# Linear attention and two expert layers on one core: the first block's four tiles scored in two pairs of batches, with quarter scores, and the last tile's state sums moved behind the first steps

## The reference, cut to what matters

```python
batch, n_heads, seq, head_dim = (4, 8, 768, 48)
for t in range(S):                         # attention, state is D x D per head
    state = alpha[:, :, t, :, None] * state + einsum('bhd,bhe->bhde', k[:, :, t], v[:, :, t])
    y[:, :, t] = einsum('bhd,bhde->bhe', q[:, :, t], state)
x = y.transpose(0, 2, 1, 3).reshape(3072, 384)
h = x @ w_in;  g = h * clip(h + 3, 0, 6) / 6;  x = g @ w_out       # 384 -> 2048 -> 384
h = x @ w_in2; g = relu(h) ** 2;               out = g @ w_out2
```

## Time and profile before

| | |
|---|---|
| median of 3 runs | 860.57 us (860.54 to 860.71) |
| the profiled execution: its time | 859.13 us |
| the profiled execution: its span | 857.4 us |
| TensorE busy | 849.5 us (99%) |
| VectorE, ScalarE, GpSimd busy | 331.1, 327.9 and 316.6 us |
| instructions | 15319 |

### The profile page before, as it was taken

The page is one execution under the profiler, slowest core; times in us unless marked ns, Lnnn a source line. Parts: engine busy times, 40 slices in busy tenths (PEclk is TensorE's granted clock), DMA queues, the critical chain, the costliest instruction groups (busy, mean ns, idle before and its releaser), DMA issues.

```text
span 857.4 us, 15319 instructions
## 1 busy us (share of the span) xinstructions
PE 849.5 (99%) x6312; PEld 703.7 (82%) x6312; DVE 331.1 (39%) x466; ACT 327.9 (38%) x586; POOL 316.6 (37%) x248
## 2 busy tenths in 40 slices
PE   8999999999999999999999999999999999999998
PEld 7888888888888888888888888888888888888886
DVE  8977545564455555421333311212211211211111
ACT  4754433343434333333445423333323333323332
POOL 2855443344433443433333333333333333333332
PEclk9999999999999999999999999999999999999999
DMA  9743233332233332200323001000000000100101
GB/s 351 296 108 96 40 95 87 90 78 72 71 81 100 86 80 75 61 16 5 111 74 111 0 1 38 1 0 26 12 1 8 29 1 0 37 1 1 37 0 39
DMA packets 67496, 51.84 MB, mean 60 GB/s; under 512 B 50785, under 2 KB 57185, under 8 KB 67425
## 3 DMA queue, kind: packets, MB, share of 16 engines
q1 hardware_dynamic: 67424, 50.84, 19.4%
HBM read 40.60 MB, written 8.26 MB: 57 GB/s over the span
## 4 chain that ended last, share of the span: by engine, by line
PE 97%; DMA 1%; SPq 0%; ACT 0%; issue 0%; ACTq 0%
PE h_ps L1046 46%; PE o_ps L1059 46%; PE att_all L939 1%; PE att_all L923 1%; DMA w_in_raw<-w_in 1%; PE att_all L990 1%; PE att_all L1014 1%; SPq L400 0%; PE h_ps L976 0%; ACT k_tok L561 0%; PE att_all L901 0%; PE att_all L976 0%; SPq L406 0%; SPq L402 0%; ACT squares L549 0%
## 5 line engine op out<-in xcount | busy, mean ns | idle before, releaser
L522 POOL TENSOR_TENSOR g_parts<-h_act,g_parts 128x512 fp32r<-128x512 f32 x192 | 257.8, 1343 | 518.9 <-ACT g_parts L603 518.8
L1059 PE MATMUL o_ps<-g_parts,w_out_hi 128*128 128x512 f32 x1152 | 327.0, 389 | 0.0
L1046 PE MATMUL h_ps<-x_parts,w_in_hi 128*128 128x512 f32 x1152 | 295.3, 392 | 0.0
L1059 PEld LDWEIGHTS o_ps<-g_parts,w_out_hi 128*128 128x128 f32 x1152 | 216.1, 188 | 45.0 <-POOL g_parts L522 0.2
L1046 PEld LDWEIGHTS h_ps<-x_parts,w_in_hi 128*128 128x128 f32 x1152 | 214.4, 188 | 45.3
L603 ACT ACTIVATE g_parts<-h_act 128x512 fp32r<-128x512 f32 x192 | 121.3, 632 | 271.4 <-PE o_ps L1059 241.5
L787 DVE SCALAR_TENSOR_TENSOR h_act<-h_ps,h_gate 128x512 f32<-128x512 f32 x96 | 66.3, 691 | 290.5 <-ACT h_gate L598 290.5
L1059 PE MATMUL o_ps<-g_parts,w_out_lo 128*128 128x512 f32 x576 | 165.6, 389 | 0.0
L1046 PE MATMUL h_ps<-x_parts,w_in_lo 128*128 128x512 f32 x576 | 161.7, 389 | 0.0
L1046 PEld LDWEIGHTS h_ps<-x_parts,w_in_lo 128*128 128x128 f32 x576 | 108.1, 188 | 22.6
L1059 PEld LDWEIGHTS o_ps<-g_parts,w_out_lo 128*128 128x128 f32 x576 | 108.1, 188 | 22.5
(11 more groups left out here) (114 smaller groups left out, 375.8 us busy)
## 6 DMA issues: line engine op xcount, KB each, us to landing
inputs<-att_in SPq DMA_DIRECT2D x18, 772.0 KB, 4.5
w_in_raw<-w_in SPq DMA_DIRECT2D x8, 768.0 KB, 7.8
w_out_raw<-w_out SPq DMA_DIRECT2D x8, 768.0 KB, 9.1
result<-inputs SPq DMA_DIRECT2D x18, 256.0 KB, 2.4
inputs<-v_in SPq DMA_DIRECT2D x20, 192.0 KB, 2.8
k_tok<-turned_keys SPq DMA_DIRECT2D x18, 192.0 KB, 2.9
x_mid<-att_in SPq DMA_DIRECT2D x4, 772.0 KB, 8.9
turned_keys<-x_mid SPq DMA_DIRECT2D x36, 64.0 KB, 2.3
```

Source lines behind the costliest of these rows:

```text
L522: nc.gpsimd.tensor_tensor(g_parts[:, g % 2, 1, :], h_act[:, g % 2, :], g_parts[:, g % 2, 0, :].bitcast(F32), ALU.subtract).then_inc(g_lo, 1)
L1046: last = nc.tensor.matmul(h_ps[g % 2][:, :], w[:, m, cols], x_parts[:, n % 2, part, m, :], start=m == 0 and i == 0, stop=m == KT - 1 and i ...
L1059: return nc.tensor.matmul(o_ps[m][:, :], w[:, f, m * P:(m + 1) * P], g_parts[:, g % 2, part, :], start=f == 0 and w is w_out_hi and part = ...
```

## The change

Only the first block's attention is changed, and the order of the work up to step 3.

- `score` writes quarters: early keys by early queries, late keys by late queries, and early keys by late queries (the "cross" part, which needs no mask). Two batches share one table: batch b of a pair goes to PSUM rows 64b to 64b + 63. A tile has 24 products of 64 columns where it had 16 of 128 (each is two instructions in the trace).
- `mask(p)` masks a pair of tiles at once with two instructions of 512 columns, one for the early quarters, one for the late ones, instead of two for each tile. ScalarE copies the cross part to SBUF (`copy_cross`).
- `attend_first(p)` multiplies a pair's values in products of 64 x 64 by 64 columns: three early shares of 8 products, six late ones.
- All four keys are scaled by GpSimd, directly after the first scan of their tile. `split_w(0)` follows on GpSimd with no wait for the queries.
- `first_state` is one copy of 112 rows instead of two of 48. The values for the state sums come as a further input, four transfers of 192 KB.
- ScalarE's `split_w(1)` moves behind the last tile's results and `copy_keys(3)`. `add_up_first(3)` moves to step 3, and `first_state(3)` too. The clearing of `state`, the full mask and the last two groups of dummy matmuls go.

```diff
-WARM_UP = (14, 8, 3, 2)
+WARM_UP = (14, 8)
 @@ SP
             load_tile(1)
+            load_tile(2)
+            load_values_to_sum(0)
+            load_tile(3)
             load_values(0)
-            load_tile(2)
             load_values(1)
-            load_tile(3)
             load_w(0)
+            load_values_to_sum(1)
+            load_values_to_sum(2)
             load_values(2)
             load_values(3)
             load_w(1)
+            load_values_to_sum(3)
 @@ GpSimd
-            for t in (1, 2):
-                pool.wait_ge(to_token_made, t + 1)
+            for t in range(BATCH):
                 scale_keys(t)
-            pool.wait_ge(q_scaled, BATCH)
             split_w(0)
             split_w(1)
 @@ ScalarE
             check_to_token(0)
-            x_high(0)
+            copy_cross(0)
+            copy_keys(1)
             first_state(0)
-            split_w(0)
-            copy_keys(1)
             check_from_end(1)
             check_to_token(1)
+            x_high(0)
             x_high(1)
+            split_w(0)
+            copy_keys(2)
             first_state(1)
-            copy_keys(2)
-            split_w(1)
-            copy_keys(3)
-            x_high(2)
+            first_state(2)
+            copy_cross(1)
             for m in range(KT):
                 last_x_high(m)
-            first_state(2)
-            first_state(3)
+            copy_keys(3)
+            split_w(1)
             check_from_end(2)
 ...
+                if g == score_at(BATCH):
+                    first_state(BATCH - 1)
 @@ VectorE
             make_decays(0)
-            scale_keys(0)
             scale_queries(0)
             make_decays(1)
+            scale_queries(1)
+            make_from_end(2)
             mask(0)
-            scale_queries(1)
-            make_decays(2)
-            mask(1)
+            make_to_token(2)
             scale_queries(2)
             make_decays(3)
-            scale_keys(3)
             scale_queries(3)
-            mask(2)
-            mask(3)
-            for t in range(BATCH - 1):
+            mask(1)
+            for t in range(2):
                 x_low(t)
 @@ TensorE
+                early, late = slice(PART, TILE), slice(0, PART)
+                for keys_of, first_query, place, signal in ((early, 0, FIRST_SCORES, None),
+                                                            (late, PART, [c + SCORES_W for c in FIRST_SCORES], scored),
+                                                            (early, PART, FIRST_CROSS, cross_scored)):
+                    ...
+                            last = nc.tensor.matmul(banks[PART * b:PART * (b + 1), col:col + PART], keys(t)[rows, j, keys_of],
+                                                    queries(t)[rows, j, first_query:first_query + PART], ...)
 ...
             warm_up(1)
-            attend_first(0)
-            add_up_first(0)
             score(1)
             turn_keys(1)
-            warm_up(2)
-            attend_first(1)
+            add_up_first(0)
+            attend_first(0)
             add_up_first(1)
             score(2)
             turn_keys(2)
-            pe.wait_ge(masked, 2)
-            warm_up(3)
             add_up_first(2)
             score(3)
+            attend_first(1)
             turn_keys(3)
-            attend_first(2)
-            attend_first(3)
-            add_up_first(3)
 ...
+                if g == score_at(BATCH):
+                    add_up_first(BATCH - 1)
```

More of the change, by code:

```diff
@@ L140, in hi_parts @@
 def hi_parts(t):
[L143 removed]
+    return t + 1 if t < 2 else 2 + KT + 2 * (t - BATCH + 1)
 def pieces_of(t):
@@ L328, in chunked_program @@
         v_loaded = [sem(f"v_loaded{i}") for i in range(BATCH + 2)]
+        vs_loaded = [sem(f"vs_loaded{i}") for i in range(BATCH)]
         w_loaded = [sem(f"w_loaded{i}") for i in range(len(W_ORDER))]
@@ L585, in first_state @@
                 act.wait_ge(u_made, t + 1)
-                act.wait_ge(state_cleared, 1)
-                for half in range(2):
-                    rows = half_rows(half)
-                    nc.scalar.activation(state[rows, t, :, :], sums(t, half), ACT.Copy).then_inc(state_made, 1)
+                nc.scalar.activation(state[:, t, :, :], first_sums(t), ACT.Copy).then_inc(state_made, 2)
             def gate(g):
@@ L896, in score @@
-                for j in range(PAIRS):
-                    for part in range(2):
-                        cols = slice(HALF * part, HALF * (part + 1))
-                        for half, bank in enumerate((bank_even, bank_odd)):
-                            rows = half_rows(half)
-                            last = nc.tensor.matmul(bank[cols, j * TILE:(j + 1) * TILE], keys(t)[rows, j, cols],
-                                                    queries(t)[rows, j, :], start=True, stop=True)
-                            if j == PAIRS - 1 and part == 1:
-                                last.then_inc(scored, 1)
+                past(pe, masked, 4 * p)
@@ new lines, in attend_first @@
+            def attend_first(p):
+                pe.wait_ge(masked, 4 * p + 2)
+                if p:
+                    pe.wait_ge(state_made, 6)
+                for m in FIRST_ORDER[p]:
+                    if p and m == 0:
+                        pe.wait_ge(cross_copied, 2)
+                    if p and m == 2:
+                        pe.wait_ge(masked, 8)
+                    share(p, m, 0, 2 * p, masked_first[:, :, 0:PAIRS, :], True)
+                pe.wait_ge(cross_copied, p + 1)
+                pe.wait_ge(masked, 4 * p + 4)
+                for m in range(KT):
+                    share(p, m, 1, 2 * p, cross_scores, True)
+                    last = share(p, m, 1, 2 * p + 1, masked_first[:, :, PAIRS:, :], False)
+                    if p and m < KT - 1:
@@ L980, in attend_first @@
                         last.then_inc(last_y_made, 1)
-                last.then_inc(y_made, 1)
+                last.then_inc(y_made, 2)
             def attend(t):
```

215 lines of the change are left out of this document (117 added, 98 removed).

## The result

The kernel after took 870.26 us (median of 6 runs, 867.79 to 871.31), the one before 860.64 us in the same sessions (6 runs, 860.54 to 861.19). The ratio is 1.0108, with a 95% interval of 1.0094 to 1.0121: slower by 9.6 us where 5.5 was forecast, and 1.7 above the range. The profiled execution has a span of 868.9 us against 857.4, so 11.5 us of difference are in the trace to be found.

The account below looks back on a forecast made before the run. The prediction took the time as the start of `hidden(0)` plus a TensorE stream without holes. Its terms, 2.9 + 2.2 + 0.4 = +5.5 us, gave 864.6 profiled, 866.1 as median, range 861.7 to 868.6.

Parts of the forecast that it names:

- parts 1 and 2: VectorE and GpSimd before `hidden(0)`: GpSimd's keys delay second scans; its first split delays tile 3's queries to 24.4, not 21.0.
- The walk of VectorE: Forecast timeline of VectorE's scans, masks and query scalings through tiles 0 to 3, tile 3's second scan ending at 20.4.
- The waiting engine wins: At the SBUF port shared by VectorE and GpSimd, GpSimd's waiting split goes before tile 3's query scaling: 3.4 us taken.
- Rival B: Tile 3's query scaling keeps its place ahead of GpSimd's split; `hidden(0)` at 25.7, median 862.7; chance 0.25.
- rival C: The VectorE-GpSimd port is no bar in these tiles; `hidden(0)` at 24.7, holes about 0, 859.5, not slower; chance 0.20.
- part 3: TensorE from tile 3's scaled queries through scores, masks, attention and turned keys: `hidden(0)` at 29.1 against 26.21, +2.9 us.
- T: The start of `hidden(0)`, the first step: 26.21 us in the kernel before, forecast 29.1.
- Rival D: TensorE idles from 20.7 to 24.5 and its clock falls; four microseconds at half rate, +1, 867.1; chance 0.10.
- Part 4: Steps behind `hidden(0)`: late `split_w(1)` delays GpSimd's second split and `low(1)`, so TensorE waits; holes of +2.2 us.
- Part 5: `add_up_first(3)` placed in step 3 adds 0.35 us and two switches of shape: +0.4 us, 0.56 at most.

Follow-up runs that it names:

- e9: Kernel before, with GpSimd no longer waiting for tile 3's query scaling ahead of its first split; 868.75 us.
- e1: Kernel after, with GpSimd's first split waiting again until all four queries are scaled; 870.61 us.
- e4: Kernel after with 3 dummy products of 512 columns ahead of `score(2)` and 11 of 128 behind `add_up_first(2)`; 871.31 us.
- e5: e2 with its 14 and 8 dummy products of 128 columns replaced by 4 and 2 of 512; 867.75 us.
- e12: e3 with 3 dummy products of 512 columns ahead of `score(2)`; 870.21 us.
- e10: Kernel before without its 3 dummy products ahead of tile 1's attention and 2 ahead of tile 2's sums; 862.25 us.
- e7: Kernel after with the loads held after tile 3's values until TensorE has turned tile 2's keys; 868.29 us.
- e2: Kernel after with ScalarE's `split_w(1)` moved early, ahead of `copy_cross(1)`; 865.99 us.
- e3: Kernel after with both the edit of e1 and that of e2; 867.22 us.
- e11: Kernel before with ScalarE's second split moved behind the state copies of tiles 2 and 3; 865.57 us.
- e16: e14 with each group's late share right behind its merged product, and nothing left out of the sums; 863.90 us.
- e8: Kernel before with its 14, 8, 3 and 2 dummy products of 128 columns replaced by 56, 32, 12 and 8 of 32; 896.10 us.
- e13: e3 with products that share weights merged: early keys against all 128 queries, early values against both parts; 864.96 us.
- e14: e2 with products that share weights merged: early keys against all 128 queries, early values against both parts; 863.98 us.

## Why the prediction was wrong

**Direction and parts 1 and 2: right in themselves.** Slower was forecast at 0.75. The walk of VectorE, the second scans of 2.1 to 2.2 us and the query scaling (23.8 to 24.4 forecast, ended 24.6) came as written. The waiting engine wins: the split made the scaling 3.74 us long in the kernel after, and in e9 two splits together made TensorE stand still for 5.5 us. Rival B's mechanism (the scaling keeps its place) and rival C (the port is no bar) are refuted by these two traces. But in the changed kernel those 3.4 us were not on the path. e1 took them away and the time stayed. So that `hidden(0)` came late was forecast from a delay that set nothing there, and this half of the right direction is luck.

**The step that failed is part 3, "from queries to T": +2.9 forecast, +6.0 measured.** It priced 48 instructions by their durations, and those held: 48 records in 1.6 us at the high clock. It had TensorE through with its own work and idle from 20.7 us, waiting for the query scaling, and did not ask where the instructions come from. 588 records stand ahead of T instead of 358, and each block of 126 waits for a packet behind a full data queue. The hole of 2.45 us at record 347 and the low clock from it on made TensorE arrive at tile 3's scores at 25.74, 1.1 us behind the scaling, and half rate took most of the rest of the way to T. The holes of e4, e5 and e12 (at 220 or 221, 346 or 347, 472 or 473, and 599 or 600), e10 (the same hole in the kernel before) and e7 (sooner packets, a shorter hole) show that it is the instruction supply. How T's 3.1 us divide between hole and clock is not shown, since what e12 saved on the clock it lost to the next packet. No rival had the supply. The rows for it existed: the packets at 15.9, 22.3 and 28.6 us in the trace of before, and a count of 358 in the earlier trace rows.

**Rival D was mis-sized.** It did happen, but at the issue hole and not in a wait for the queries. It was priced at 4 us of half rate and +1. The clock was low for some 10 us ahead of `hidden(0)`, and the work in it (rest of the scores, turned keys, sums, tile 3's scores, first attention: 1.55 + 1.01 + 0.89 + 2.83 + 1.72 = 8.0 us) takes 0.92 + 0.60 + 0.56 + 1.61 + 1.06 = 4.75 at the high clock (rows of e2 and e4): an estimate of 3.2 us. In e12, against e3, T came 1.9 us earlier without it, and the next packet took that back. It came a second time behind the wait for `low(1)`, which D did not have.

**Part 4: the mechanism right, the size short.** The second split began at T + 2.3 (forecast 2.2) and TensorE waited for `low(1)` (forecast 1.5, measured 2.60). The holes were put at +2.2. With the low clock behind the wait, `hidden(0)` to `hidden(5)` took 5.4 us more, where +2.2 and +0.4 were forecast. The wait of 2.60, half of the 3.4 us of low clock from 47.6, the hole of 0.29 and some 0.5 of tile 3's sums make 5.1 of them. Taking the late split away returned 4.3 us (e2). The late split in the kernel before cost 4.9 us as a median (e11), with its mechanism seen only in part.

**Part 5** was measured only beside the low clock: the sums took 0.88 us at half rate against 0.56. Whether +0.4 was right stays open. Open too are the 3.2 us that the best version (e16, 863.9) still lies above the kernel before. Its trace, of the slowest of its five runs (865.1), starts `hidden(0)` 3.8 us late, with a hole of 0.92 us at record 221, 1.66 us of waiting for masks and 3.4 us of low clock in it; behind it TensorE waits 1.36 us for `low(1)`, though the second split is over by 28.8.

## What to carry to other kernels

Count instructions as well as durations where TensorE works through many small products while loads fill the DMA queues: here it got 126 matmuls with their weight loads per 6 to 7 us, and a hole put down to "issue" at a fixed count from the start is the sign. Merging products that share their weights was worth 5.6 us by itself and 2.0 beside the early split: faults that cover each other do not add up. A wait between two engines that share a port can be what protects the path (one line, 8.1 us), and a short pause of TensorE must be priced with the slow stretch that can follow it.

## What was not expected of the hardware

- Instruction packets of 16 KB came 6.0 to 7.0 us apart beside a full data queue in the kernels before and after, e4 and e5, and once 9.3 us (e10). When the loads were held back (e7), one came 4.3 us behind another.
- With 32 records fewer early the first packet came late (16.2 us in e5 against 12.5 in e2), and the median was 1.8 us higher.
- Dummy products with 128 x 128 weights and 32 columns took 0.21 us each, and a TensorE filled with them ran at the lower clock, by the durations, to about 46 us (e8).
- The length of a pause did not tell whether the clock falls. Pauses of 1.35 and 0.85 us were followed by none of it (e10: 1.00 from 6 to 26.2 us), but one of 1.38 us in the same trace was, at 42.5. The hole of 2.45 us had the drop inside it, 1 us after its start, in the kernel after; in e2, with the same hole, the drop came 1.8 us behind its end, inside the next pause of 0.63 us. One of 1.66 us was followed by 3.4 us of low clock in e13 and e16 and by none in e14.
